# Seven filler matmuls around the third attention unit's scores in a one-core attention, MLP and expert kernel

## What is computed

```python
q_d = q.reshape(B, H, Sd, factor, D).mean(axis=3)     # the same for k_d, v_d; factor = 4, Sd = 144
out_d = sm_attn(q_d, k_d, v_d)
out_up = np.repeat(out_d, factor, axis=2)
mask = np.abs(pos[:, None] - pos[None, :]) < factor
scores = np.where(mask, scale * np.matmul(q, k.transpose(0, 1, 3, 2)), -1000000000.0)
...
return (out_up + out_local).astype(np.float32)
```

## Time and profile before

| | |
|---|---|
| median of 3 runs | 1096.08 us |
| lowest and highest | 1094.14 and 1102.39 us |
| profiled execution, its own time | 1100.69 us |
| its span | 1098.1 us |
| PE busy | 1083.3 us (99%) |
| DVE busy | 599.3 us (55%) |
| ACT busy | 415.0 us (38%) |
| mean granted clock of PE | 0.986 |

### The profile page before, as it was taken

The page is one execution under the profiler, slowest core; times in us unless marked ns, Lnnn a source line. Parts: engine busy times, 40 slices in busy tenths (PEclk is TensorE's granted clock), DMA queues, the critical chain, the costliest instruction groups (busy, mean ns, idle before and its releaser), DMA issues.

```text
span 1098.1 us, 17856 instructions
## 1 busy us (share of the span) xinstructions
PE 1083.3 (99%) x6994; PEld 992.4 (90%) x6994; DVE 599.3 (55%) x1052; ACT 415.0 (38%) x671; POOL 25.7 (2%) x32
## 2 busy tenths in 40 slices
PE   8999999999999999999999999999999999999998
PEld 4779999999998988998998899899889889989987
DVE  4686665556557864644455364455446536444542
ACT  2447654344324531432342153234225314323421
POOL 3220000000000000000000000000000000000000
PEclk7799999999999999999999999999999999999999
DMA  7372111322130210220130031022002102200111
GB/s 190 108 210 78 44 57 55 90 84 63 58 111 20 86 50 1 73 64 20 32 101 19 0 96 38 19 57 76 19 19 80 45 8 60 74 19 21 36 38 48
DMA packets 30225, 64.98 MB, mean 59 GB/s; under 512 B 12396, under 2 KB 14700, under 8 KB 30188
## 3 DMA queue, kind: packets, MB, share of 16 engines
q1 hardware_dynamic: 30188, 64.47, 19.6%
HBM read 62.10 MB, written 2.36 MB: 59 GB/s over the span
## 4 chain that ended last, share of the span: by engine, by line
PE 95%; DVE 2%; DMA 1%; issue 1%; ACT 1%; SPq 0%
PE ps L1145 57%; PE ps L1429 32%; PE ps L1172 1%; PE ps L1226 1%; PE ps L1221 1%; DMA kt<-kT 1%; PE ps L1190 1%; DVE x_lo L716 0%; PE ps L1201 0%; PE ps L1185 0%; PE ps L1238 0%; PE ps L1166 0%; DVE mx L723 0%; DVE xf L915 0%; DVE e_t L727 0%
## 5 line engine op out<-in xcount | busy, mean ns | idle before, releaser
L1145 PE MATMUL ps<-w_hi,h_hi 128*128 128x512 f32 x576 | 224.4, 390 | 0.0
L1145 PE MATMUL ps<-w_lo,h_hi 128*128 128x512 f32 x576 | 224.2, 389 | 0.0
L1145 PE MATMUL ps<-w_hi,h_lo 128*128 128x512 f32 x576 | 224.2, 389 | 0.0
L643 ACT ACTIVATE h_hi<-h 128x1024 fp32r<-128x1024 f32 (+1 forms) x80 | 77.3, 975 | 238.1 <-PE ps L1145 217.3
L1429 PE MATMUL ps<-x_hi,w_hi 128*128 128x288 f32 x512 | 151.5, 296 | 1.9 <-DVE x_lo L716 1.9
L1429 PE MATMUL ps<-x_hi,w_lo 128*128 128x288 f32 x512 | 151.5, 296 | 0.0
L1031 DVE SCALAR_TENSOR_TENSOR acc<-ps,prob_e,acc 128x512 f32<-128x512 f32 x63 | 47.2, 750 | 190.9 <-PE ps L1145 190.9
L1429 PE MATMUL ps<-x_lo,w_hi 128*128 128x288 f32 x512 | 151.3, 296 | 0.0
L1145 PEld LDWEIGHTS ps<-w_hi,h_lo 128*128 128x128 f32 x576 | 108.1, 188 | 22.4
L1145 PEld LDWEIGHTS ps<-w_hi,h_hi 128*128 128x128 f32 x576 | 108.1, 188 | 22.1
L1145 PEld LDWEIGHTS ps<-w_lo,h_hi 128*128 128x128 f32 x576 | 108.1, 188 | 22.1
(11 more groups left out here) (134 smaller groups left out, 1728.2 us busy)
## 6 DMA issues: line engine op xcount, KB each, us to landing
raw<-w SPq DMA_DIRECT2D x64, 512.0 KB, 3.5
raw<-w_up SPq DMA_DIRECT2D x24, 512.0 KB, 3.5
raw<-w_out SPq DMA_DIRECT2D x16, 384.0 KB, 3.0
vw<-v SPq DMA_DIRECT2D x10, 252.0 KB
qt<-qT SPq DMA_DIRECT2D x4, 576.0 KB, 4.9
kt<-kT SPq DMA_DIRECT2D x4, 576.0 KB, 5.9
v<-v SPq DMA_DIRECT2D x8, 288.0 KB
out<-acc SPq DMA_DIRECT2D x9, 256.0 KB, 2.0
```

The source lines that it names most:

```text
L643: nc.scalar.activation(h2_hi[:, idx % 2, f0:f1, :], h2[:, f0:f1, t * P:(t + 1) * P], ACT.Relu).then_inc(h2_hi_ready, 1)
L1145: done = nc.tensor.matmul(dst, a, b, start=first and n == 0, stop=last and n == len(terms) - 1)
```

## The change

Seven more filler matmuls are issued by PE in step 2. Four stand ahead of the scores of unit 2, through a new test in the loop over the steps, and three behind them, through a third entry of `WARM`.

```diff
-        WARM_FIRST, WARM = 3, (2, 2)
+        WARM_FIRST, WARM = 3, (2, 2, 3)
+        GAP_STEP, WARM_GAP = 2, 4
...
             for s in steps:
+                if s == GAP_STEP:
+                    warm(WARM_GAP)
                 if is_unit(s):
                     unit_scores(s)
                 if s < len(WARM):
```

## The result

| | before | changed |
|---|---|---|
| median | 1097.22 us (22 executions) | 1095.28 us (22 executions) |
| lowest to highest | 1094.14 to 1102.52 | 1091.08 to 1096.91 |
| profiled execution's span | 1098.1 us | 1092.3 us |
| its mean granted clock | 0.986 | 0.995 |
| ratio of changed to before | | 0.9972, 95% interval 0.996 to 0.9985 |

By the ratio the kernel is about 3.1 us faster (0.28% of 1097.2), by the medians 1.9 us, against the 6.3 us forecast. The time, 1095.28, lies in the range, and within 1% of before, but the gain is a little less than half of the one worked out. In the two profiled executions, though, the spans lie 5.8 us apart. That is the first thing to explain.

What follows compares the result with a forecast made beforehand. PE was taken to set the pace at half clock from 17 to 40 us, then DVE's chain. 2.9 us lost, 10.5 won back, 1.3 lost: 6.3 us faster, 1089.8 us, range 1086 to 1097.

Steps and rivals of the forecast that it cites:

- Step 1: Fillers around unit 2's scores: they first delay unit 1's transposes from 17.16 to 20.1, costing 2.9 us.
- Step 2: PE from unit 1's transposes to 33.3 us: full clock wins back 10.5 us, leaving 7.6 us net.
- Step 3: DVE's earlier chain meets POOL's unmoved second-batch value sums: between nothing and 2.6 us given back, 1.3 taken.
- the first meeting in full and the second as today: DVE's x_lo beside POOL's two sums: first loses up to 1.3 us, second today's 1.08; 1.3 us extra charged.
- I take the gain off the median: Whole kernel: 6.3 us subtracted from the runs' median 1096.1, not the profiled execution's 1100.7, giving 1089.8 us.
- the sum's own bounds: Whole kernel: gain of 4.0 to 7.6 us, so 1092.1 to 1088.5; with 2 us of median error, 1086.5 to 1094.
- the later fall: Rival: the clock still falls, about unit 1's values or in kernel steps 4 or 5; 1095 us, chance 0.21.
- a clock of 0.50 anywhere before 33: Sign in the changed profile, before 33 us, that would show the forecast wrong; it expected 1.00 from 17 to 34.
- Slower, only a delay: Rival: the clock falls before about 20 us, so the fillers' 2.9 us delay stays; 1099.0 us, chance 0.08.

Runs made afterwards that it cites:

- clean picture: Profiled execution of the changed kernel run again unedited, clock 1.00 up to 343 us: span 1093.0 us; that run's median 1095.22 us, ratio 0.9978.
- The cut sums: POOL's first value sum cut into four instructions, a quarter of the columns each, against the changed kernel: ratio to before 0.9956, median 1094.08 us.
- before's second profile: Profiled execution of the kernel before, run again unchanged: span 1099.2 us; that run's median 1097.11 us, ratio 0.9999.
- before with cut sums: The kernel before with POOL's first value sum in quarters and no new fillers: ratio 0.9996, median 1098.27 us; profiled span 1091.2 us.

## Why the prediction was right and wrong

- **Step 1, the fillers' cost: right.** Forecast 16.7 and 20.1 for unit 2's scores and unit 1's transposes, measured 16.72 and 20.04 in the clean picture. At equal mean clock the changed kernel is slower by about this delay: at 0.995 the span of before has a median of 1090.6 (4 executions), that of the changed kernel 1093.5 (11 executions), 2.9 us more; at 0.994 it is 3.1 us and at 0.997 2.7 us.
- **Step 2, full clock: right as a mechanism.** Step 4 forecast at 24.4, measured 24.48; step 7 at 33.3, measured 33.28.
- **Step 3, POOL: mis-sized.** I took "the first meeting in full and the second as today, 1.3 us". In the clean picture both were paid in full: DVE's seven steps took 24.27 us (37.34 to 61.61) in place of 21.81, so 2.5 us. The MLP starts 5.1 us earlier in the clean picture (62.53 against 67.64): 7.6 less 2.5. By the Trainium skill's page "SBUF — State Buffer", section "SBUF: two separate sides", the loser of the lock waits for the other's whole instruction. This trace agrees: x_lo ends 0.26 and 0.27 us after POOL's sum (39.23 against 38.97, 49.03 against 48.76). The cut sums agree as well. The row at 48.85 had shown it before; I should have let it decide. But "as today" had no one value either: before lost 1.1 us in one profile and 2.7 in the other, the changed kernel 2.2 and 3.6. What this term is in the median execution is open.
- **"I take the gain off the median": the step that failed.** It took the low stretch of one profiled execution as that of each. The profiled span of before, 1098.1, lay 2.4 us above the median of 109 (1095.7). The clean gain of 5.1 us less those 2.4 is 2.7; the medians of the spans differ by 2.25 (1095.7 and 1093.45, 34 executions of the changed kernel). Between before's second profile and the clean picture the spans differ by 6.2 us, nearly the forecast: the sum was good for such an execution, and most are not like it. The forecast's 4.6 us between profiled execution and median stood in the text as a distance to subtract from, not as a sign that the executions differ in just the thing the change removes.
- **That the time lies in the range is luck.** By the sum's own bounds it should have been at most 1094. The upper end of 1097 stood there for the later fall, which did not come. Part of the distance from 1089.8 is the baseline: the median of 3 runs was 1096.1, that of 22 is 1097.2.
- **The later fall** did not come: 17 to 34 us held 1.00 in both profiles of the changed kernel, with the small down units and their transposes in it. The Trainium skill says in "TensorE: Matmul & The Clock Gate", section "Part 4: PE-mode transpose", that transposes don't count as PE being busy in the same way. That stretch does not bear it out. The sign "a clock of 0.50 anywhere before 33" did appear, at 7.7 to 11, but ahead of the new fillers, and the second profile of before has it too (0.53).
- **Slower, only a delay:** this rival holds for part of the executions. 13 of 109 executions of before lie at 0.994 or above, with spans of 1089.4 to 1092.6, under the changed kernel's median. In such executions the fillers can win little, and at an equal mean clock the changed kernel takes some 2.9 us more (step 1).

What stays open: the time outside the span is 2.5 us on average in before and 1.8 in the changed kernel, and nothing here says why. Those 0.7 us are part of the 3.1. And what decides in which executions the clock comes back early was not shown; no experiment could set it. The cause of the smaller gain is shown by the spans and clocks of many executions; that it is the stretch of 17 to 40 us which varies among them rests on three profiles.

## What to carry to other kernels

If the granted clock falls in a profile, look at the clock of many executions ahead of pricing a cure by one: the cure wins only what the typical execution loses. Fill a gap ahead of PE with as many matmuls as it holds, and look first whether filling an earlier one closes it as well; the surplus here cost about 1 us, which is inside the noise. Then look what the surplus had covered. When one engine's work moves earlier, lay it beside the work of the engine that did not move, instruction by instruction.

## What was not expected of the hardware

After some 6 us of unbroken work at 0.50 the clock came back in the profile of before with cut sums (17 to 23.2, above), and after 23 us it had not in that of before itself, with the same PE instructions; what made the difference is not shown. One program's mean clock ranged from 0.984 to 0.997, with its span from 1100.7 to 1089.4 us. And four instructions of 0.72 us each in place of one of 2.35 on POOL were 0.4 us longer in all, yet let DVE in between.
